# A sparse attention, routed experts and mixer kernel: six wait places on VectorE moved, and a chain of nested conditional blocks written side by side

## What is computed

```python
scores = scale * np.matmul(q, k.transpose(0, 1, 3, 2))
kth = np.partition(scores, -32, axis=-1)[..., -32:-31]
scores = np.where(scores >= kth, scores, -1000000000.0)
attn = np.exp(scores - np.max(scores, axis=-1, keepdims=True))
attn = attn / (np.sum(attn, axis=-1, keepdims=True) + 1e-09)
x = np.matmul(attn, v)                       # (4, 8, 576, 64)
...
e = fresh_e if s == 0 or local_gate[b, s] < 0.5 else prev_e
out[b, s] = p[e] * (np.maximum(x[b, s] @ w1[e], 0.0) @ w2[e])
...
mixed = np.real(np.fft.fft(np.fft.fft(x, axis=1), axis=2))
u = x + mixed
un = (u - mu) / np.sqrt(var + 1e-06)
return u + np.maximum(un @ w_ch1, 0.0) @ w_ch2
```

## Time and profile before

| | |
|---|---|
| median of three runs | 1504.94 us |
| the profiled execution's own time | 1504.39 us |
| its span, first to last instruction | 1502.5 us |
| TensorE matmul busy | 1374.4 us (91%) |
| VectorE busy | 1050.8 us (70%) |
| ScalarE, GpSimd busy | 596.7 us, 612.9 us |
| mean granted TensorE clock | 0.937 |
| attention | 0 to about 740 us |
| routing | about 740 to 763 us |
| experts | 763 to 984 us |
| mixer | 984 to 1502 us |

### The profile page before, as it was taken

How to read it: one execution, slowest core, us unless ns; L and a number is a source line. 1 busy time by engine, 2 the same in 40 slices (tenths; PEclk the granted TensorE clock), 3 DMA queues, 4 the chain that set the end, 5 groups by cost and what they waited for, 6 DMA issues and landing times. The chain is left out here.

```text
span 1502.5 us, 23125 instructions
## 1 busy us (share of the span) xinstructions
PE 1374.4 (91%) x7974; PEld 1129.0 (75%) x7974; DVE 1050.8 (70%) x2158; ACT 596.7 (40%) x1596; POOL 612.9 (41%) x493
## 2 busy tenths in 40 slices
PE   6889899899779999999679999957999999999998
PEld 4677677677557766777469999925777899999987
DVE  7999999999989999999855444536653522422221
ACT  4545555555426556555224433413312211311211
POOL 3666666666746776777213344302220200000000
PEclk9989998989969999999879999957999999999999
DMA  3101111011263342442506457133321111311111
GB/s 116 33 26 34 33 34 33 9 33 32 89 231 108 105 159 97 166 134 71 188 29 234 156 212 263 49 134 119 113 70 47 58 59 42 127 43 43 42 43 63
DMA packets 74992, 138.09 MB, mean 92 GB/s; under 512 B 27443, under 2 KB 27572, under 8 KB 74882
## 3 DMA queue, kind: packets, MB, share of 16 engines
q1 hardware_dynamic: 52602, 74.65, 15.2%
q10 hardware_dynamic: 13352, 35.03, 6.5%
q0 software_dynamic: 8928, 27.00, 5.1%
HBM read 108.35 MB, written 30.42 MB: 92 GB/s over the span
## 5 line engine op out<-in xcount | busy, mean ns | idle before, releaser
L655 POOL TENSOR_SCALAR keep<-s_sb,top 128x576 f32<-128x576 f32 x142 | 244.6, 1722 | 218.7 <-DVE top L682 218.5
L682 DVE MAX8 top<-w_sb 128x8 f32<-128x576 f32 x432 | 306.8, 754 | 0.0
L391 PEld LDWEIGHTS ps_o<-v_sb,eT 128*128 128x128 f32 (+1 forms) x1440 | 190.8, 194 | 59.8 <-issue 47.5
L1748 DVE SCALAR_TENSOR_TENSOR h_lo<-ps_ch,h_hi 128x384 fp32r<-128x384 f32 x96 | 53.5, 557 | 242.3 <-ACT h_hi L1599 242.3
L391 PE MATMUL ps_o<-v_sb,eT 128*128 128x74 f32 (+3 forms) x1440 | 216.8, 289 | 0.0
L684 DVE MATCH_REPLACE8 w_sb<-top,w_sb 128x576 f32<-128x576 f32 x288 | 212.8, 750 | 0.0
L659 POOL TENSOR_TENSOR e_sb<-e_sb,keep 128x576 f32<-128x576 f32 x142 | 200.1, 1409 | 25.2 <-ACT e_sb L529 4.0
L1599 ACT ACTIVATE h_hi<-ps_ch 128x384 fp32r<-128x384 f32 x96 | 47.1, 491 | 286.2 <-PE ps_ch L1431 286.2
L363 PE MATMUL ps_t<-ident,e_sb 128*128 128x128 f32 x576 | 102.5, 305 | 61.5 <-POOL e_sb L659 50.8
L1429 PE MATMUL ps_ch<-un_hi,w_hi 128*128 128x384 f32 x384 | 132.0, 344 | 1.6 <-DVE un_lo L1742 1.6
L518 ACT ACTIVATE eT<-ps_t 128x512 f32<-128x512 f32 x144 | 86.1, 598 | 113.1 <-PE ps_t L363 100.6
(11 more groups left out here) (315 smaller groups left out, 2410.7 us busy)
## 6 DMA issues: line engine op xcount, KB each, us to landing
w<-in_w ACTq DMA_DIRECT2D x16, 2048.0 KB, 8.1
w<-in_w SPq DMA_DIRECT2D x12, 2048.0 KB, 11.0
stage<-in_w_ch SPq DMA_DIRECT2D x16, 512.0 KB, 3.3
q_sb<-in_q SPq DMA_DIRECT2D x16, 288.0 KB, 2.8
vT<-in_vt SPq DMA_DIRECT2D x16, 288.0 KB, 3.1
x_d<-rows SPq DMA_DIRECT2D x18, 256.0 KB, 5.4
u<-u_d SPq DMA_DIRECT2D x18, 256.0 KB, 2.7
x_d<-u POOLq DMA_DIRECT2D x18, 256.0 KB, 2.6
```

The lines of the kernel that those rows point to most:

```text
L391: mm = pe.matmul(ps_o[k % 2][:, lo:hi], eT[k % NT_][0:n, c, :], v_sb[b][0:n, c, lo:hi], start=(c == 0), stop=(c == KC))
L655: pool.tensor_scalar(keep[t % 2][:, :], s_sb[t % NS][:, :], top[t % NS][:, TOPK - 1:TOPK], None, ALU.is_ge).then_inc(s_keep, 1)
L682: dve.max(eight, src).then_inc(s_top, 1)
```

## The change

First, four of the six places in `AWAIT` move forward, by 2, 3, 3 and 3 operations. The places where TensorE does its side, `HOPS`, stay.

Second, in `blocks` the conditions of blocks 12 to 24 no longer stand within each other but one behind the other. With 25 possible blocks, every engine now tests all 13 of them, whatever the number used. What is in a body does not change. The lines behind this place move up by five (L1103 becomes L1101, L1164 becomes L1159, L1177 becomes L1172).

```diff
-    AWAIT = [(ROUTE + n, at) for n, at in ((0, 9), (1, 0), (1, 9), (1, 13), (2, 3), (3, 7))]
+    AWAIT = [(ROUTE + n, at) for n, at in ((0, 9), (1, 0), (1, 7), (1, 10), (2, 0), (3, 4))]
...
             for j in range((SURE - 2) // 2 * 2, SURE):
                 body(j // 2, j % 2)
-
-            def rest(j):
-                if j < NBLK:
-                    with eng.If(used > j):
-                        body(j // 2, j % 2)
-                        rest(j + 1)
-
-            rest(SURE)
+            for j in range(SURE, NBLK):
+                with eng.If(used > j):
+                    body(j // 2, j % 2)
```

## The result

Over 20 runs of each kernel on the same chips the changed kernel took 1516.68 us in the median (1512.60 to 1527.22) and the kernel before 1507.19 us (1503.32 to 1517.89). The ratio is **1.0055**, with a 95% interval of 1.0035 to 1.0075: slower by half a per cent. Against the profiled execution of before that is 1.0055 x 1504.39 = 1512.7 us; the profiled execution of the changed kernel took 1512.85 us, its span is 1511.0 us. The forecast was 1512.3 us.

What follows compares the result with a forecast made beforehand. VectorE was taken to bound the attention, TensorE the experts, and the latest engine the seam to the mixer. The sum was 1504.39 - 1.4 + 9.3 = 1512.3 us, with 1503 to 1520 for 8 in 10.

Steps and rivals of the forecast that it cites:

- part two: End of experts: TensorE's nine jumps wait for code pieces one by one, arriving at 993.2 instead of 977.2; +9.3 us.
- Rival one: TensorE's jumps: no piece is waited for, GpSimd decides the barrier; 1504.8 us, down to 1501.7; chance 0.18.
- Rival two: TensorE's jumps: each costs the exit's 3.67 us; 1525.7 us; chance 0.11, shared with more pieces at a higher price.
- Part one: AWAIT places in the attention: the last at_pos comes earlier and the chain behind follows; -1.4 us, ends -3.1 and 0.
- Three of them are 2.1 us: VectorE before the last at_pos: three fewer 14-a-pair operations stand ahead of it, 0.66 + 0.73 + 0.73 us.
- 1.33 us lost: VectorE at L127: it waits for L81 and goes on two MAX8 behind, 397.99 - 396.66 us.
- rival three: VectorE's new waits not swallowed, L87 or L415 slipping from 0.8 us on; 1513.7 to 1514.7 us; chance 0.13.
- Earlier places can miss one of these or both: Small VectorE operations stretched beside GpSimd's L659: missing one gains 1.1 us more, both 2.3 us more.
- All of that chain is behind L769: TensorE's gates, ScalarE's weight loads and score copies, and VectorE's wait all move with L769; 1.4 us earlier.
- The 1.33 us lost is swallowed by the 4.91 us wait: VectorE in the attention: time lost at L127 disappears in its later 4.91 us wait for scores until 437.73.
- step one: The forecast for the AWAIT places in the attention: 1.4 us earlier, with 0 and 3.1 as the ends.
- if that wait ends at 437.7 or later: VectorE's wait for L538, forecast to end at about 436.3 us; ending this late would refute the AWAIT forecast.

Runs made afterwards that it cites:

- the run of this part alone: Kernel before with only the four AWAIT places moved, conditions still nested: 1503.94 us against 1505.95, ratio 1.0006 [0.9984, 1.0028].
- the last experiment: Kernel before with the second expert's weight loads issued two tiles later, plus the changed kernel's AWAIT: 1502.32 us in one run.

## Why the prediction was right

**The direction, the mechanism and the size of part two** were right. The forecast was that TensorE enters the pieces one after another and waits for each: six pieces, the first already on its way, five to be asked for, one fetch to each. The trace has six long jumps; the first, 1.6 us long, ends at 975.55 (forecast 975.2), and the five others take 16.1 us with the short ones between, 3.2 us apiece instead of 3.5. TensorE arrives at 992.1 (forecast 993.2). GpSimd's hops were to cost 1.8 us and be covered; the run without TensorE's chain puts them at 1.2 us, and they are covered. The seam grew by 7.3 us, not 9.3. Five pieces at 0.3 us less are 1.4, less the 0.35 us by which the first ended later: TensorE was 1.1 us too early for the forecast. And the attention ended 1.0 us later than before, while TensorE's first failing test came only 0.55 us later, so that a part of the 8.3 us by which the release moved belongs to the attention. The mixer was only shifted, as assumed (518.7 us, before 518.5).

Rival one (no piece is waited for) is out by TensorE's arrival. The traced hops are 0.15 to 0.19 us on GpSimd, and on TensorE it is the pieces that cost. The 108 ns for a compare-and-branch in the Trainium skill, page "Advanced Engine Details and Errata", section "Control Flow Timing", do not give this chain's price: its nine tests took 18 us. Rival two (each jump a full miss) is out by the three jumps of 0.22 us inside the pieces at hand. The Trainium skill, page "Runtime: NRT & Kernel Launch", section "Instruction fetch mechanics", has a stall for a fetch only where the target of a taken branch is outside the two pages at hand; the short jumps agree.

**Part one was wrong in size and sign**, by about 2 us in this profile, and the two errors cancelled. Forecast -1.4 us; pair 42 came 0.8 us later, and in the run of this part alone 0.05 us later. Four steps of it, one by one:

- "Three of them are 2.1 us": right, 1.9 to 2.0 us.
- "1.33 us lost" at L127, and no wait at L133 and L733: the waits were 1.2, 1.8 and 2.1 us at L127 in three profiles. At the clock of before they come to 1.0, as forecast; the rest is L81 late by TensorE's low clock, for which the old places had 0.3 us to spare and the new ones nothing. In the changed kernel's profile rival three happened too, since TensorE at its lower clock brought L87 at 402.6, past the 0.8 us of slip I had set. Without that stretch (the part alone) rival three did not happen, and the gain was still nil: the clock is at most a part of the cause.
- "Earlier places can miss one of these or both": this is the step that failed. L769 did miss both, 2.3 us. But GpSimd's L659 still ran, and other small operations met it: L773 in both kernels with the new places, L735 and L742 too in the part alone. What is taken out of one row came back in others.
- "All of that chain is behind L769": incomplete. Once L769 comes earlier against L773, the first load waits for L778, 0.5 us.

"The 1.33 us lost is swallowed by the 4.91 us wait" was right, and the last experiment shows it from the other side. The sign I had announced as the proof against step one ("if that wait ends at 437.7 or later") is what came: it ended at 438.75.

The total of 1512.3 was 0.4 us off the 1512.7 that the ratio gives. Against the profile the steps were off by +2.2 us (part one) and -2.0 (part two), and 0.4 us are the early attention's and the mixer's own; so the closeness of the total is luck to that extent; the range of 1503 to 1520 was what the steps deserved.

## What to carry to other kernels

A chain of optional blocks belongs nested (or with one jump out), on TensorE above all: conditions side by side make the engine walk through the code of every body it skips, at 3.2 us for 16 KB here, where one jump out over six such pieces cost 3.6 to 3.9 us. The price is paid only where the engine then decides a barrier; on GpSimd it was 0.15 to 0.19 us from one test to the next, once 0.45.

A stretched row next to another engine's operation isn't a gain to be had by moving it; ask which row will stand there instead. A result that is ready 0.3 us before its use is ready only at that execution's clock: moving the use ahead gives the slack away. And a wait of the bounding engine is best followed back through the engine that releases it: here two DMA issues that stood in front of a copy were worth 5 us, more than all the reordering ahead of them.

## What the runs showed of the hardware that was not expected

- A jump beyond the next piece of code took 4.9 to 5.1 us on TensorE when it came right after another wait for a piece, and 3.6 to 3.9 us in the exits of the nested kernels.
- Some small VectorE operations beside GpSimd's L659 end only with it: L773 took 1.46 us instead of 0.24, for 96 elements in one partition. Others are not held: L127 (0.14 us) and L143 (0.23 us) ran within an L659 in the kernel before. What tells them apart was not tested.
- The first two weight loads of ScalarE took 0.4 us each to issue, the third and fourth 3.4 and 1.9 us, one behind the other (2.9 to 3.4 and 1.9 to 2.3 us in the eight profiles that issue four in a row).
- The start of pair 38 lay anywhere from 374.8 to 386.4 us in eleven profiles, although nothing differs ahead of it but the execution. Rows show short waits of VectorE and stretches of TensorE at the lower clock at other places each time. A change of a few us in this kernel is read from distances between two rows, not from the span.
